# Two fused feed-forward layers behind a window attention: in the unit that ends a layer, the matmuls of the running sums are placed ahead of those of the next product

## The chip, the cores and the metric

The kernel runs on one core of one Trainium2 chip. The metric is the device time of one execution in microseconds, lower is better. Times shown are the median of repeated executions of the same program; one further execution was taken by the hardware profiler, and everything read from a trace comes from that one.

## The reference

```python
w = weight_gen - np.max(weight_gen, axis=-1, keepdims=True)
w = np.exp(w); w = w / (np.sum(w, axis=-1, keepdims=True) + 1e-09)      # softmax over 7 taps
out = np.einsum('bshk,bskhg->bshg', w, x_unf)                           # causal window of 7 tokens, 8 heads
h = x @ w_in;  g = h * np.cos(h);            x = g @ w_out              # layer 1, 192 -> 2048 -> 192
h = x @ w_in2; g = np.maximum(0.01 * h, h);  x = g @ w_out2             # layer 2, 192 -> 2048 -> 192
```

There are 2 x 4096 tokens of 192 numbers, all in float32.

## The kernel before

**Chunks, layers and units.** The 8192 tokens are cut into 16 chunks of 512. For each chunk, layer 1 has 8 units and layer 2 has 8 units; a unit is 256 of the 2048 hidden columns. A unit has a first product (token columns times `w_in`, written into one of three PSUM buffers, the slots), then an activation by ScalarE and VectorE, which leaves the activated values as two parts, `g_hi` and `g_lo`, and then a second product (times `w_out`) that is added to two PSUM accumulators: `acc_a` holds 128 of the 192 result columns, and `acc_b` the other 64 in two halves that are added afterwards. Every factor is split in a high and a low part, so that one product is made of several matmuls.

**How TensorE is fed.** `both_products(i, q, j, r)` (L1215) puts side by side on the two halves of the array (rows 0 to 63 and rows 64 to 127) the first product of unit `q` of chunk `i` and the second product of the unit three before it, `r` of chunk `j`. These are 38 matmuls of 64 rows by 512 columns, issued as 19 pairs: one matmul of each pair on the lower half, one on the upper. Two matmuls that add to the same PSUM buffer from different halves must not overlap, so wherever a buffer changes halves there is a wait. It is for `tiles_done` within a unit, and for `summed` between the units. `summed` is counted up by the last matmul of a unit's second product. The 19 pairs of most units are: 5 pairs that only fill the slot, then, behind a wait for `g_lo` of unit `r` (`lo_ready`) and for `summed` of the unit before (L1250), 14 pairs with the sums in them. The order is written out by hand.

**The last unit of a layer.** Where `r` is the eighth unit of its layer (`v == 7` in the code, `r` 7 or 15), the order differs: `acc_b` gets its last matmul in pair 15 of 19, which counts up `summed_b`, and `acc_a` and the slot get theirs in pair 19.

**Between layers.** When the last unit is through, VectorE copies the upper half of `acc_b` to SBUF and adds the lower half to it (`fold_b` L955, `leave_mid_b` L961 for layer 1, `leave_res_b` L966 for layer 2); it waits for `summed_b`. ScalarE copies `acc_a` out (`leave_mid_a` L756, `leave_res_a` L759); it waits for `summed`. The next unit on TensorE begins the sums of the following layer: behind its 5 filling pairs it waits for both copies (`acc_a_out`, `acc_b_out`, in `wait_to_sum` L1334).

**The activation chain of a unit.** ScalarE copies the activated values to `g_hi` (L730), VectorE subtracts to get `g_lo` (L913), which counts up `lo_ready`. ScalarE's own reads of the slots and the input attention on VectorE lie between.

**Outside the steady part.** The first three units use `fill_alone` (L1352): the 5 filling pairs, a wait for `tiles_done` of the pair just before, and 4 more pairs; so do three others in the second chunk and at the end. `sum_alone` (L1372) does a second product by itself on the whole array; two of them stand right ahead of the last call of `both_products` with `r` 15.

Of the kernel before, what the change touches and what calls it, by code (L numbers as in the profile page):

```python
# [33 lines left out]
FIRST_UNITS = [0, 1, 2, 3, 4, 5, 6, 7]  # L34
# [22 lines left out]
def window_attention_two_ffn(nc, x, weight_gen, w_in1, w_out1, w_in2, w_out2, out):  # L57
# [74 lines left out]
    def unit(i, q):  # L132

        if i == 0:
            return q
        return 8 + 16 * (i - 1) + (q if i < LAST else q - 8)
# [14 lines left out]
    def first_phase(i):  # L151

        return max(0, 2 * i - 1)

    def second_phase(i):
        return 2 * i - (1 if i == LAST else 0)

    ctx = ExitStack()
    with ctx:
# [3 lines left out]
        def sem(name):  # L163
            return ctx.enter_context(nc.semaphore(name))
# [87 lines left out]
        filled = sem("filled")  # L252
        tiles_done = sem("tiles_done")
# [13 lines left out]
        summed = sem("summed")  # L267
        summed_b = sem("summed_b")
# [861 lines left out]
        def _(pe):  # L1130
# [68 lines left out]
            def row_tile_end():  # L1199

                ended[0] += 1
                return ended[0]

            def first_terms(w, x_a_hi, x_a_lo, x_b, f, half):

                c = slice(f * P, (f + 1) * P)
                return [(w.in_a_lo[:, c], x_a_hi), (w.in_a_hi[:, c], x_a_hi),
                        (w.in_a_hi[:, c], x_a_lo), (w.in_b_hi[:, b_columns(half, f)], x_b)]

            def half_product(r, to, w, x, start=False, stop=False):  # L1210

                rows = slice(r * DB, (r + 1) * DB)
                return nc.tensor.matmul(to, w[rows, :], x[rows, :], start=start, stop=stop)  # L1213

            def both_products(i, q, j, r):  # L1215

                w, x_a_hi, x_a_lo, x_b, x_up = operands(q)
                w_then = operands(r)[0]
                u, v, buf = q % 8, r % 8, r % 2
                slot = slots[UNITS[q] % SLOTS]
                P0, P1 = [slot[:, t, :] for t in range(PAIR)]
                A, B = acc_a[:, :], acc_b[:, :]
                b_lo = w.in_b_lo[:, u * P:(u + 1) * P]
                lower, upper = [[first_terms(w, x_a_hi, x_a_lo, x_b, PAIR * u + t, half)
                                 for t in range(PAIR)] for half in range(2)]
                a, b = [], []  # L1230
                for t in range(PAIR):
                    f = PAIR * v + t
                    hi, lo = [g[:, buf, t * N:(t + 1) * N] for g in (g_hi, g_lo)]
                    a_hi, a_lo, b_both = [w_then.out[:, f, c] for c in (
                        slice(0, DA), slice(DA + P, None), slice(DA, DA + P))]
                    a += [(a_hi, hi), (a_hi, lo), (a_lo, hi)]
                    b += [(b_both, hi), (b_both, lo)]

                wait_to_fill(i, q)
                for k in range(4):  # L1240
                    wait_for_tokens(i, q, k)
                    half_product(0, P0, *lower[0][k], start=k == 0)
                    half_product(1, P1, *upper[1][k], start=k == 0)
                half_product(0, P0, b_lo, x_b)
                half_product(1, P1, b_lo, x_up).then_inc(tiles_done, 1)
                first_end = row_tile_end()

                wait_to_sum(j, r)
                if unit(j, r):
                    pe.wait_ge(summed, unit(j, r))  # L1250
                for k in range(4):
                    half_product(0, B, *b[k], start=v == 0 and k == 0)
                    ins = half_product(1, A, *a[k], start=v == 0 and k == 0)
                ins.then_inc(tiles_done, 1)
                sum_b_end = row_tile_end()
                pe.wait_ge(tiles_done, first_end)
                for k in range(2):
                    half_product(0, P1, *lower[1][k])
                    ins = half_product(1, A, *a[4 + k])
                ins.then_inc(tiles_done, 1)  # L1260
                sum_a_end = row_tile_end()
                if v == len(FIRST_UNITS) - 1:
                    pe.wait_ge(tiles_done, sum_b_end)
                    for k in range(2):
                        half_product(0, P1, *lower[1][2 + k], stop=k == 1)
                        half_product(1, B, *b[k])
                    pe.wait_ge(tiles_done, sum_a_end)
                    for k in range(2):
                        half_product(0, A, *a[k])
                        ins = half_product(1, B, *b[2 + k], stop=k == 1)  # L1270
                    ins.then_inc(summed_b, 1)
                    for k in range(4):
                        sum_a = half_product(0, A, *a[2 + k], stop=k == 3)
                        fill_p = half_product(1, P0, *upper[0][k], stop=k == 3)
                    sum_a.then_inc(summed, 1)
                    fill_p.then_inc(filled, 1)
                else:
                    for k in range(2):
                        half_product(0, P1, *lower[1][2 + k], stop=k == 1)
                        half_product(1, P0, *upper[0][k])  # L1280
                    pe.wait_ge(tiles_done, sum_a_end)
                    for k in range(2):
                        half_product(0, A, *a[k])
                        ins = half_product(1, P0, *upper[0][2 + k], stop=k == 1)
                    ins.then_inc(filled, 1)
                    for k in range(4):
                        half_product(0, A, *a[2 + k])
                        ins = half_product(1, B, *b[k])
                    ins.then_inc(summed, 1)
# [19 lines left out]
            def wait_to_fill(i, q):  # L1309
                wait_for_slot(i, UNITS[q])  # L1310
                if i == 0 and q < 8:
                    piece = 0 if q < 2 else 1 if q < 5 else 2
                    pe.wait_ge(w1_hi, 2 * (piece + 1))
                    if q == 0:
                        pe.wait_ge(w1_first_lo, 2)
                    else:
                        pe.wait_ge(w1_lo, 2 * (piece + 1))
                if q == 8 and i == 1:
                    pe.wait_ge(w2_lo, len(W2_PIECES) + 1)

            def wait_for_tokens(i, q, term):

                if q == 0 and term == 0:
                    pe.wait_ge(x1_hi, i * 2 + 1)
                if q == 0 and term == 2:
                    pe.wait_ge(x1_ready, i * 2 + 1)
                if q == 0 and term == 3:
                    pe.wait_ge(x1_ready, i * 2 + 2)
                    pe.wait_ge(x1_up_ready, i + 1)
                if q == 8 and term == 0:  # L1330
                    pe.wait_ge(x2_ready, i * 2)
                    pe.wait_ge(x2_up_ready, i)

            def wait_to_sum(i, q):  # L1334
                if unit(i, q) == 0:
                    pe.wait_ge(unit_dve, 3)
                pe.wait_ge(lo_ready, unit(i, q) + 1)
                if i == 0 and q % 2 == 0:
                    pe.wait_ge(w1_out_lo, q + 2)
                if i == 1 and q >= 8 and q % 2 == 0:  # L1340
                    pe.wait_ge(w2_lo, len(W2_PIECES) + 1 + q - 8 + 2)
                if q in (0, 8) and i > 0:
                    phase = first_phase(i) if q == 0 else second_phase(i)
                    pe.wait_ge(acc_a_out, phase)
                    pe.wait_ge(acc_b_out, phase)

            def operands(q):
                if q < 8:
                    return W1, x1_a_hi, x1_a_lo, x1_b, x1_up
                return W2, x2_a_hi, x2_a_lo, x2_b, x2_up  # L1350
# [29 lines left out]
            def iteration(i):  # L1380
                for q in range(LAG):
                    both_products(i, q, i - 1, q - LAG + len(UNITS))
                for q in range(LAG, len(UNITS)):
                    both_products(i, q, i, q - LAG)
# [25 lines left out]
            for q in range(LAG, 8):  # L1410
                both_products(0, q, 0, q - LAG)
# [47 lines left out]
```

## Time and profile before

| what | value |
|---|---|
| median of 3 executions | 1144.72 us (1144.63 to 1144.95) |
| the profiled execution, its own time | 1145.67 us |
| its span (first to last instruction) | 1143.9 us |
| TensorE matmuls (PE) busy | 1129.4 us, 99% of the span |
| TensorE weight loads (PEld) busy | 996.5 us, 87% |
| VectorE (DVE) busy | 932.0 us, 81% |
| ScalarE (ACT) busy | 723.1 us, 63% |
| GpSimd (POOL) busy | 88.8 us, 8% |
| mean granted TensorE clock | 0.999 |

PE is the matmul side of TensorE, PEld its weight loads, which run beside the matmuls. The start of a matmul is recorded; its end is modelled. Two matmuls of a pair start a few hundredths of a microsecond apart, and each is recorded as 0.39 us long while a new pair starts every 0.227 us, so a busy share of 99% includes overlaps, and small delays have to be read from the distance between starts, not from idle time.

### The profile page before, as it was taken

Reading aid. Unit: us, or ns where it says so; the run is one execution under the profiler, and the core shown is the slowest. Engines: PE = TensorE matmul, PEld = TensorE weight load, DVE = VectorE, ACT = ScalarE, POOL = GpSimd, SP = SyncE. Lnnn points to the kernel's source line nnn. Section 1 sums busy time; section 2 is a strip of 40 time slices with the busy share of each in tenths; the row PEclk is TensorE's granted clock in tenths of the full one; section 3 lists DMA queues with packets and bytes.
Section 4 is the critical chain, followed back from the end, with each engine's and each line's share of the span. In section 5 each row is a group of like instructions: output and inputs, shape, how many; then the busy total and the mean of one; then the engine's idle time right before and its main releaser. Section 6 shows DMA issues by size and latency. Waiting matters only on the chain.

```text
span 1143.9 us, 22933 instructions
## 1 busy us (share of the span) xinstructions
PE 1129.4 (99%) x9766; PEld 996.5 (87%) x9766; DVE 932.0 (81%) x911; ACT 723.1 (63%) x775; POOL 88.8 (8%) x82
## 2 busy tenths in 40 slices
PE   7999999999999999999999999999999999999998
PEld 5778888888988888898888988889899998988986
DVE  7999897988979899697896969879797896978443
ACT  6766775757657576574755757566575655757544
POOL 6860000000000000000000000000000000000000
PEclk9999999999999999999999999999999999999999
DMA  9760201102011110301103011020201102010001
GB/s 256 209 127 1 63 1 40 38 14 64 1 42 36 31 48 1 77 1 36 43 1 77 1 39 40 15 63 1 59 20 32 46 1 77 1 38 6 1 15 29
DMA packets 85262, 48.41 MB, mean 42 GB/s; under 512 B 58156, under 2 KB 78762, under 8 KB 84776
## 3 DMA queue, kind: packets, MB, share of 16 engines
q1 hardware_dynamic: 80712, 41.70, 14.3%
q0 software_dynamic: 4448, 5.24, 2.4%
q8 instruction: 77, 1.26, 0.5%
q14 instruction: 25, 0.20, 0.1%
HBM read 35.12 MB, written 11.80 MB: 41 GB/s over the span
## 4 chain that ended last, share of the span: by engine, by line
PE 91%; DVE 3%; ACT 1%; issue 1%; ACTq 0%
PE slot L1213 42%; PE acc_a L1213 29%; PE acc_b L1213 18%; DVE g_lo L913 1%; DVE gate L1027 1%; ACT gate L793 0%; PE acc_b L1186 0%; PE acc_a L1179 0%; PE acc_b L1187 0%; PE acc_a L1178 0%; PE acc_a L1177 0%; DVE x_a_lo L941 0%; ACT g_hi L730 0%; ACT taps_w L856 0%; DVE gate L908 0%
## 5 line engine op out<-in xcount | busy, mean ns | idle before, releaser
L1213 PE MATMUL acc_a<-g_hi,out_hi_lo 64*128 64x512 f32 x2000 | 696.3, 388 | 0.0
L913 DVE TENSOR_TENSOR g_lo<-gate,g_hi 128x1024 fp32r<-128x1024 f32 x251 | 307.9, 1227 | 121.5 <-ACT g_hi L730 121.4
L1213 PEld LDWEIGHTS acc_a<-g_hi,out_hi_lo 64*128 64x128 f32 x2000 | 367.8, 184 | 26.1
L1213 PE MATMUL acc_b<-g_hi,out_hi_lo 64*128 64x512 f32 x1000 | 388.4, 388 | 1.3 <-DVE g_lo L913 1.2
L1213 PE MATMUL acc_a<-g_lo,out_hi_lo 64*128 64x512 f32 x1000 | 386.5, 386 | 0.0
L1213 PE MATMUL acc_b<-g_lo,out_hi_lo 64*128 64x512 f32 x1000 | 386.4, 386 | 0.0
L730 ACT ACTIVATE g_hi<-gate 128x1024 fp32r<-128x1024 f32 x251 | 266.2, 1061 | 107.7 <-PE acc_b L1213 86.0
L1213 PE MATMUL slot<-x_a_hi,in_a_lo 64*128 64x512 f32 x1024 | 301.0, 388 | 1.6 <-DVE g_lo L927 1.2
L1213 PE MATMUL slot<-x_b,in_b_hi 64*128 64x512 f32 x1024 | 300.6, 387 | 0.5 <-DVE x_b L951 0.2
L1213 PE MATMUL slot<-x_a_lo,in_a_hi 64*128 64x512 f32 x1024 | 300.3, 387 | 0.0
L1213 PE MATMUL slot<-x_a_hi,in_a_hi 64*128 64x512 f32 x1024 | 300.1, 386 | 0.0
L793 ACT ACTIVATE gate<-slot 128x1024 f32<-128x1024 f32 x128 | 130.7, 1021 | 121.6 <-PE slot L1213 95.4
L1213 PEld LDWEIGHTS acc_b<-g_hi,out_hi_lo 64*128 64x128 f32 x1000 | 184.0, 184 | 18.8 <-issue 6.1
L1213 PEld LDWEIGHTS acc_a<-g_lo,out_hi_lo 64*128 64x128 f32 x1000 | 184.2, 184 | 12.0
L1213 PEld LDWEIGHTS acc_b<-g_lo,out_hi_lo 64*128 64x128 f32 x1000 | 184.1, 184 | 9.9
L1027 DVE SCALAR_TENSOR_TENSOR gate<-slot,whole 128x1024 f32<-128x1024 f32 x127 | 155.1, 1221 | 42.4 <-ACT whole L789 41.6
L789 ACT ACTIVATE whole<-slot 128x1024 int32<-128x1024 f32 x127 | 129.9, 1023 | 65.4 <-PE slot L1213 65.4
L1213 PEld LDWEIGHTS slot<-x_a_hi,in_a_lo 64*128 64x128 f32 x1024 | 145.6, 184 | 17.2 <-PE slot L1213 3.0
L1213 PEld LDWEIGHTS slot<-x_b,in_b_hi 64*128 64x128 f32 x1024 | 145.8, 184 | 13.7 <-DVE x_b L944 1.1
L1213 PEld LDWEIGHTS slot<-x_a_lo,in_a_hi 64*128 64x128 f32 x1024 | 145.7, 184 | 12.5 <-DVE x_a_lo L948 0.3
L1213 PEld LDWEIGHTS slot<-x_a_hi,in_a_hi 64*128 64x128 f32 x1024 | 145.7, 184 | 11.6
L908 DVE SCALAR_TENSOR_TENSOR gate<-slot,gate 128x1024 f32<-128x1024 f32 x123 | 150.4, 1223 | 6.1 <-ACT gate L830 4.2
(110 smaller groups left out, 1023.8 us busy)
## 6 DMA issues: line engine op xcount, KB each, us to landing
x_win<-in_x SPq DMA_DIRECT2D x14, 960.0 KB, 4.8
x_columns<-prods SPq DMA_DIRECT2D x56, 96.0 KB, 2.0
out<-turned_a SPq DMA_DIRECT2D x240, 16.0 KB, 1.5
x_raw_a<-x_columns SPq DMA_DIRECT2D x14, 256.0 KB, 2.9
out<-turned_b SPq DMA_DIRECT2D x120, 16.0 KB, 1.5
result<-x_columns SPq DMA_DIRECT2D x14, 128.0 KB, 3.0
out_raw<-in_moe_w_out SPq DMA_DIRECT2D x3, 512.0 KB, 9.7
out_hi_lo<-in_moe_w_out POOLq DMA_DIRECT2D x2, 768.0 KB, 10.2
```

Of the source, the lines that this page charges most:

```text
L730: nc.scalar.activation(g_hi[:, q % 2, :], result_of(i, q), ACT.Copy)\
L789: nc.scalar.activation(whole[:, q % 2, :], slot, ACT.Identity, bias=0.25)\
L793: nc.scalar.activation(gate[:, q % 2, :], slot, ACT.Prelu, alpha=0.01)\
L908: nc.vector.scalar_tensor_tensor(result_of(i, q), slot, RADIANS, gate[:, q % 2, :], ALU.mult, ALU.mult).then_inc(g_ready, 1)
L913: nc.vector.tensor_tensor(g_lo[:, q % 2, :], result_of(i, q), g_hi[:, q % 2, :].bitcast(FP32), ALU.subtract)\
L1027: nc.vector.scalar_tensor_tensor(gate[:, q % 2, :], slot, 0.25, whole[:, q % 2, :], ALU.add, ALU.subtract)\
L1213: return nc.tensor.matmul(to, w[rows, :], x[rows, :], start=start, stop=stop)
```

## The change

In `both_products`, where `r` is the last unit of a layer and not the very first such unit (`unit(j, r) > 7`), another order of the same 38 matmuls is used, and the function returns. There are 30 such calls. The sums' first 4 pairs come first, behind the waits for `lo_ready` and for `summed` of the unit before; then the 5 filling pairs; then 4 pairs with sums alone, of which the last ends `acc_b` (pair 13); then 6 mixed pairs. `acc_a` and the slot still get their last matmul in pair 19. Nothing else is changed: VectorE's, ScalarE's, GpSimd's and the DMA queues' programs are the same row for row.

```diff
+                if v == len(FIRST_UNITS) - 1 and unit(j, r) > v:
+                    wait_to_sum(j, r)
+                    pe.wait_ge(summed, unit(j, r))
+                    for k in range(4):
+                        half_product(0, B, *b[k])
+                        ins = half_product(1, A, *a[k])
+                    ins.then_inc(tiles_done, 1)
+                    sums_end = row_tile_end()
+                    wait_to_fill(i, q)
+                    for k in range(4):
+                        wait_for_tokens(i, q, k)
+                        half_product(0, P0, *lower[0][k], start=k == 0)
+                        half_product(1, P1, *upper[1][k], start=k == 0)
+                    half_product(0, P0, b_lo, x_b)
+                    half_product(1, P1, b_lo, x_up).then_inc(tiles_done, 1)
+                    first_end = row_tile_end()
+                    pe.wait_ge(tiles_done, sums_end)
+                    for k in range(4):
+                        half_product(0, A, *a[k])
+                        ins = half_product(1, B, *b[k], stop=k == 3)
+                    ins.then_inc(summed_b, 1)
+                    pe.wait_ge(tiles_done, first_end)
+                    for k in range(2):
+                        half_product(0, A, *a[4 + k])
+                        ins = half_product(1, P0, *upper[0][k])
+                    ins.then_inc(tiles_done, 1)
+                    sum_a_end = row_tile_end()
+                    for k in range(2):
+                        half_product(0, P1, *lower[1][k])
+                        half_product(1, P0, *upper[0][2 + k], stop=k == 1)
+                    pe.wait_ge(tiles_done, sum_a_end)
+                    for k in range(2):
+                        fill_p = half_product(0, P1, *lower[1][2 + k], stop=k == 1)
+                        sum_a = half_product(1, A, *a[4 + k], stop=k == 1)
+                    sum_a.then_inc(summed, 1)
+                    fill_p.then_inc(filled, 1)
+                    return
```

The first place is TensorE's queue at the start of the last unit of layer 1 in the second chunk (`slot1` is the slot being filled; words in brackets are semaphores that the matmul's weight load waits for). Before:

```order
L1213 MATMUL acc_a<-g_lo,out1_hi_lo 128x512
L1213 MATMUL acc_b<-g_hi,out1_hi_lo 128x512
L1213 MATMUL acc_a<-g_hi,out1_hi_lo 128x512
L1213 MATMUL acc_b<-g_lo,out1_hi_lo 128x512
L1213 MATMUL slot1<-x2_a_hi,in2_a_lo 128x512 [waits g_ready]
L1213 MATMUL slot1<-x2_a_hi,in2_a_lo 128x512
L1213 MATMUL slot1<-x2_a_hi,in2_a_hi 128x512 x2
L1213 MATMUL slot1<-x2_a_lo,in2_a_hi 128x512 x2
L1213 MATMUL slot1<-x2_b,in2_b_hi 128x512 x2
L1213 MATMUL slot1<-x2_b,in2_b_lo 128x512
L1213 MATMUL slot1<-x2_up,in2_b_lo 128x512
L1213 MATMUL acc_b<-g_hi,out1_hi_lo 128x512 [waits summed,lo_ready]
```

In the changed kernel the same place reads:

```order
L1213 MATMUL acc_a<-g_lo,out1_hi_lo 128x512
L1213 MATMUL acc_b<-g_hi,out1_hi_lo 128x512
L1213 MATMUL acc_a<-g_hi,out1_hi_lo 128x512
L1213 MATMUL acc_b<-g_lo,out1_hi_lo 128x512
L1213 MATMUL acc_b<-g_hi,out1_hi_lo 128x512 [waits summed,lo_ready]
L1213 MATMUL acc_a<-g_hi,out1_hi_lo 128x512
L1213 MATMUL acc_b<-g_lo,out1_hi_lo 128x512
L1213 MATMUL acc_a<-g_lo,out1_hi_lo 128x512
L1213 MATMUL acc_b<-g_hi,out1_hi_lo 128x512
L1213 MATMUL acc_a<-g_hi,out1_hi_lo 128x512
L1213 MATMUL acc_b<-g_lo,out1_hi_lo 128x512
L1213 MATMUL acc_a<-g_hi,out1_hi_lo 128x512
```

The wait for `summed` and `lo_ready` stood five pairs behind the matmul that counts `summed` up, and now stands directly behind it.

The second place is TensorE's queue around the last matmul of `acc_b` in the same unit, from there to the unit's end. Before:

```order
L1213 MATMUL acc_a<-g_lo,out1_hi_lo 128x512
L1213 MATMUL acc_b<-g_lo,out1_hi_lo 128x512
L1213 MATMUL acc_a<-g_hi,out1_hi_lo 128x512
L1213 MATMUL slot1<-x2_a_hi,in2_a_lo 128x512
L1213 MATMUL acc_a<-g_hi,out1_hi_lo 128x512
L1213 MATMUL slot1<-x2_a_hi,in2_a_hi 128x512
L1213 MATMUL acc_a<-g_lo,out1_hi_lo 128x512
L1213 MATMUL slot1<-x2_a_lo,in2_a_hi 128x512
L1213 MATMUL acc_a<-g_hi,out1_hi_lo 128x512
L1213 MATMUL slot1<-x2_b,in2_b_hi 128x512
```

In the changed kernel:

```order
L1213 MATMUL acc_b<-g_lo,out1_hi_lo 128x512
L1213 MATMUL acc_a<-g_lo,out1_hi_lo 128x512 [waits tiles_done]
L1213 MATMUL slot1<-x2_a_hi,in2_a_lo 128x512
L1213 MATMUL acc_a<-g_hi,out1_hi_lo 128x512
L1213 MATMUL slot1<-x2_a_hi,in2_a_hi 128x512
L1213 MATMUL slot1<-x2_a_hi,in2_a_lo 128x512
L1213 MATMUL slot1<-x2_a_lo,in2_a_hi 128x512
L1213 MATMUL slot1<-x2_a_hi,in2_a_hi 128x512
L1213 MATMUL slot1<-x2_b,in2_b_hi 128x512
L1213 MATMUL slot1<-x2_a_lo,in2_a_hi 128x512 [waits tiles_done]
L1213 MATMUL acc_a<-g_lo,out1_hi_lo 128x512
L1213 MATMUL slot1<-x2_b,in2_b_hi 128x512
```

Behind the last matmul of `acc_b` there were 4 pairs to the unit's end, and now there are 6 (the first block ends with the unit; of the second only the closing `acc_a` matmul is left out). The next unit's rows are the same in both: 5 filling pairs, then the matmul that waits for `acc_b_out`, `acc_a_out`, `summed` and `lo_ready`.

## Rows read from the trace of the kernel before

**Rows 1.** The page: busy time of each engine (us, share of span, instructions)

```profile
PE 1129.4 (99%) x9766; PEld 996.5 (87%) x9766; DVE 932.0 (81%) x911; ACT 723.1 (63%) x775; POOL 88.8 (8%) x82
```

**Rows 2.** The windows view: stretch, then busy us per engine, granted clock, DMA

```profile
64.60:1095.80 1031.20, 1030.10 (x9040) 921.43 (x9036) 857.92 (x824) 660.08 (x697) 44.98 (x38) 1.00 0.13 31
```

**Rows 3.** The timeline, TensorE, from a middle unit into a last one (start, length)

```profile
308.18 0.39 PE L1213 MATMUL acc_b<-g_lo,out_hi_lo 64*128 64x512 f32 x1
308.35 0.44 PE L1213 MATMUL slot<-x_a_hi,in_a_lo 64*128 64x512 f32 x2
```

**Rows 4.** The timeline, TensorE's matmuls, inside a unit that only fills (near the end)

```profile
1108.79 0.39 PE L1213 MATMUL slot<-x_b,in_b_lo 64*128 64x512 f32 x1
1108.79 0.39 PE L1213 MATMUL slot<-x_up,in_b_lo 64*128 64x512 f32 x1
1109.25 0.50 PE L1213 MATMUL slot<-x_a_hi,in_a_lo 64*128 64x512 f32 x2
1109.59 0.39 PE L1213 MATMUL slot<-x_a_hi,in_a_hi 64*128 64x512 f32 x2
```

**Rows 5.** The timeline, TensorE's weight loads, same place (in brackets: idle before, releaser)

```profile
1109.25 0.19 PEld L1213 LDWEIGHTS slot<-x_a_hi,in_a_lo 64*128 64x128 f32 x2 [0.50 <-PE slot L1213]
1109.36 0.19 PEld L1213 LDWEIGHTS slot<-x_a_hi,in_a_hi 64*128 64x128 f32 x2
```

**Rows 6.** The timeline, VectorE: g_lo of two last units

```profile
272.42 1.22 DVE L913 TENSOR_TENSOR g_lo<-gate,g_hi 128x1024 fp32r<-128x1024 f32 x1
...
305.45 1.23 DVE L913 TENSOR_TENSOR g_lo<-gate,g_hi 128x1024 fp32r<-128x1024 f32 x1
```

**Rows 7.** The timeline, TensorE, the start of the last unit at 273.77

```profile
273.56 0.39 PE L1213 MATMUL acc_b<-g_lo,out_hi_lo 64*128 64x512 f32 x1
273.77 0.40 PE L1213 MATMUL slot<-x_a_hi,in_a_lo 64*128 64x512 f32 x2
```

**Rows 8.** The timeline around 1101, last call with r 15: TensorE, then VectorE

```profile
1101.01 0.50 PE L1213 MATMUL slot<-x_a_hi,in_a_lo 64*128 64x512 f32 x2
1101.35 0.40 PE L1213 MATMUL slot<-x_a_hi,in_a_hi 64*128 64x512 f32 x2
...
1100.42 1.23 DVE L913 TENSOR_TENSOR g_lo<-gate,g_hi 128x1024 fp32r<-128x1024 f32 x1
```

**Rows 9.** The timeline, between the layers at 312: all engines

```profile
312.10 0.69 DVE L958 COPY fold<-acc_b 64x512 f32<-64x512 f32 x1 [0.76 <-PE acc_b L1213]
...
312.65 0.44 PE L1213 MATMUL slot<-x_a_hi,in_a_lo 64*128 64x512 f32 x2
...
312.83 0.68 DVE L963 TENSOR_TENSOR mid_b<-acc_b,fold 64x512 f32<-64x512 f32 x1
312.85 0.60 ACT L757 ACTIVATE mid_a<-acc_a 128x512 f32<-128x512 f32 x1 [3.13 <-PE acc_a L1213]
...
317.07 0.41 PE L1213 MATMUL slot<-x_a_hi,in_a_lo 64*128 64x512 f32 x2
```

**Rows 10.** The timeline, behind layer 2 at 486: VectorE, ScalarE, TensorE

```profile
486.18 0.85 DVE L976 TENSOR_TENSOR res_b<-acc_b,fold 64x256 f32<-64x256 f32 x2
...
486.34 0.60 ACT L764 ACTIVATE res_a<-acc_a 128x512 f32<-128x512 f32 x1 [1.82 <-PE acc_a L1213]
...
486.15 0.40 PE L1213 MATMUL slot<-x_a_hi,in_a_lo 64*128 64x512 f32 x2
...
490.57 0.44 PE L1213 MATMUL slot<-x_a_hi,in_a_lo 64*128 64x512 f32 x2
```

**Rows 11.** The waits: who waited for whom, us in total, times, longest

```profile
DVE fold L958 <- PE acc_b L1213: 26.0, 30, 3.1
PEld acc_b L1213 <- issue: 6.1, 29, 0.5
```

**Rows 12.** The timeline, TensorE, the slowest start of a layer's sums

```profile
174.44 0.39 PE L1213 MATMUL slot<-x_b,in_b_lo 64*128 64x512 f32 x1
...
174.96 0.46 PE L1213 MATMUL acc_b<-g_hi,out_hi_lo 64*128 64x512 f32 x1
```

## The prediction

> **What bounds the kernel now.** I read the page first. TensorE's matmuls are busy for 99% of the span, VectorE for 81%, ScalarE for 63% [rows 1]. The windows view says the same of the steady part alone: from 64.6 to 1095.8 us PE is busy for 1030.10 of 1031.20 us at a granted clock of 1.00, the upper of its two levels, 2.4 GHz [rows 2]. So the time is the number of pairs times the distance between their starts, plus the places where that distance is longer. Since ends of matmuls are modelled, idle time does not show these places, and I went to the timeline and measured starts. A pair follows the one before after 0.227 us, and a unit of 19 pairs takes 4.30 us: in rows 3 a last unit starts at 308.35 and in rows 9 its successor starts at 312.65. A change that only reorders matmuls can therefore gain no more than the delays that stand in the timeline now, and it loses whatever it adds to the distance between two pairs.
>
> **What the change can gain.** Each layer's sums start behind a wait for the two copies of the old accumulators. In rows 9 ScalarE's copy of `acc_a` runs from 312.85 to 313.45, VectorE's work on `acc_b` ends at 312.83 + 0.68 = 313.51, so `acc_b` is the last by 0.06 us. The unit that waits there takes 317.07 - 312.65 = 4.42 us, which is 0.12 over a plain unit. Behind layer 2 `acc_b` is through at 486.18 + 0.85 = 487.03 and `acc_a` at 486.94 [rows 10]; that unit takes 490.57 - 486.15 = 4.42 us, again 0.12 over. The waits view counts 29 such starts, where the weight load of the first sum stood idle for 6.1 us in all [rows 11]. That idle time is an upper figure, since part of it is there without any wait; 29 times 0.12 is 3.5 us, and this is what I take as the delay.
>
> The new order ends `acc_b` two pairs earlier, 2 x 0.227 = 0.45 us. VectorE can use it: it was idle 26.0 us ahead of its 30 copies of `acc_b`, 0.87 us each on the mean and 0.76 in rows 9 [rows 9, 11]. So `acc_b` stops being the last. What is late next is `acc_a`. Its last matmul stays in pair 19, ScalarE's copy still takes 0.60 us, and it ends only 0.06 to 0.09 us ahead of today's last. I take that 0.07 of the 0.12 goes and 0.05 stays. One start was slower than the others: the first sum came 174.96 - 174.44 = 0.52 us behind the last filling pair instead of 0.227 [rows 12], and with 0.45 us more cover I expect nearly all of the extra 0.3 to go. The gain is 29 x 0.07 + 0.3, some **2.3 us**. Its bounds are nothing (if `acc_a` alone sets these starts) and 29 x 0.12 + 0.3 = 3.8 us (if all delays go).
>
> **What the change costs.** The new first matmul of a last unit waits for `summed` of the unit before. That semaphore is counted up by the very matmul that now stands directly ahead of it, where before five filling pairs, 1.13 us, lay between and hid it. On TensorE everything queues behind that weight load, the filling pairs too, and both halves of the array run dry. The kernel of before has the same pattern in one place: a unit that only fills waits for the pair just issued. There the pair starts at 1108.79 and ends at 1109.18, and the next weight load and its matmul start at 1109.25 [rows 4, 5]. That is 0.46 us from start to start in place of 0.227. The pair behind it also comes late, at 1109.59, 0.34 us on, because its weights could only be loaded from 1109.36 [rows 5]; of the 0.34, 0.227 is the plain distance. So one such wait costs (0.46 - 0.227) + (0.34 - 0.227) = 0.23 + 0.11 = **0.34 us**. In rows 4 the two matmuls of the pair start together. In rows 3 the second starts at 308.18, 0.06 behind the first (308.35 - 0.227 = 308.12), so its end and the semaphore would come 0.06 later, and the price is 0.39 to 0.40. In rows 7 the same reckoning gives only 0.02. Since a drained array starts both halves together, I take 0.34 for all.
>
> There are 30 calls. In 29 of them nothing else is later: `g_lo` of the last unit, now wanted 1.13 us earlier, is ready at 305.45 + 1.23 = 306.68 where the unit starts at 308.35 [rows 3, 6]. In the tightest place that I found it is ready at 272.42 + 1.22 = 273.64, while the `summed` wait lets the load go only at about 273.56 + 0.39 + 0.06 = 274.01, where 0.06 is the distance from the modelled end to the load in rows 4 and 5 [rows 4 to 7]. So 29 x 0.34 = **9.9 us**. The thirtieth is the last call, at 1101.01. There the preceding matmuls run on the whole array, and `g_lo` is only ready at 1100.42 + 1.23 = 1101.65 [rows 8]. The unit would start at about 1101.71 instead of 1101.01, with the same 0.34 to the second pair as now, so it adds **0.7 us**; half of it might be given back by later waits, and a rather later start costs 0.9.
>
> The three waits for `tiles_done` within the new unit lie five, four and two pairs behind what they wait for. Today's lie four and two behind (the code at L1215 and below), and the last unit that starts in rows 3 takes the plain 4.30 us with them in it, so they cost nothing. The filling pairs and their wait for a free slot come 4 pairs later, which can only relax it. The slot is filled in pair 19 as before, so ScalarE's and VectorE's next reads keep their distance. Every TensorE delay gives these engines slack, and they have the same rows to do.
>
> **The sum.** 9.9 + 0.7 - 2.3 = **+8.3 us**. Against the profiled execution, 1145.67 us, that is 1154.0; the median of the runs shown is 0.95 lower, and against it I say **1153.0 us**. The bounds: 29 x 0.33 + 0.4 - 3.8 = +6.2 and 29 x 0.40 + 0.9 - 0 = +12.5, so 1150.9 to 1157.2. About 0.2%, 2.3 us, is what a measurement of this kernel tells from no change, and the change is well over it.
>
> **The rivals.** *Faster: the new wait is hidden.* Break-even is at (2.3 - 0.7) / 29 = 0.055 us per wait. If the queue covered the `summed` wait to less than that, only the gain would be left: 1144.72 - 2.3 + 0.7 = 1143.1, or 1142.4 without the late `g_lo`. For it: the same `summed` wait costs nothing in all units now. Against it: there five pairs stand between, and where none does the trace shows 0.34 us [rows 4]. Chance 0.04.
>
> *Half price: the second pair is not late.* If the second pair's weights were in place when the first may start, the 0.11 would fall away: 29 x 0.23 + 0.7 - 2.3 = +5.1, so 1149.8. Against it: rows 4 and 5 show the second pair's load starting 0.11 behind the first's. Chance 0.06. The Trainium skill, page "TensorE: Matmul & The Clock Gate", section "Part 2: What happens when you issue a matmul", says that TensorE may pull weight loads ahead of matmuls in flight where the row groups don't conflict; by that rule the upper half's load would not stand behind the lower half's wait, and the sum would come out nearer this rival. This trace shows the loads of both halves held until the wait ends [rows 5], and I go by the row.
>
> *More: other waits appear.* Each layer change holds TensorE up for a third of a microsecond, and the activation chain may fall out of step so that `g_lo` is late in some of the 29, by up to the 0.7 of the last call. If it were in every third, 10 x 0.7 more, +15, some 1160. Against it: a delay on TensorE leaves this chain's work the same and its time longer. Chance 0.06.
>
> *No change within the bound.* It needs the new wait at about 0.05 to 0.1 us and the whole gain; 1144.7. Chance 0.03.
>
> **How the numbers follow.** The forecast has 0.81. The range takes its bounds and the half-price rival's neighbourhood: 1150.4 to 1157.2. Faster by over 0.2%: 0.04; within: 0.03; slower: 0.93.
>
> **What would show it.** Right: in the timeline, at the 30 last units the first sum's pair starts 0.45 to 0.46 us behind the pair before and the next one 0.34 us on; the waits view has a new row of about 29 waits of `acc_b`'s weight load for PE, some 0.5 us of idle each; last units take 4.64 us. `fold` starts about 0.45 us earlier against the end of its unit, `acc_b`'s copy ends before `acc_a`'s, and units behind a layer change take 4.35 rather than 4.42 us. Wrong: last units at 4.30 us (first rival), at 4.53 (second), or a row of `acc_b`'s weight load waiting for `g_lo` with more than a few entries (third).

## The result, and the profile after

The changed kernel is **slower**: 1155.95 us (median of 6, 1155.28 to 1156.38) against 1144.88 us (median of 6), a ratio of 1.0096 with a 95% interval of 1.0086 to 1.0106. That is 11.1 us. The prediction said 1153.0 us and a range up to 1157.2. The two profiled executions lie 10.3 us apart (spans 1143.9 and 1154.2 us), since the one of before took 0.8 us more than its median. All executions compared below ran at a granted clock of 0.998 or more; one of summed_on_load ran at 0.557 and took 1910.78 us, and the ratios leave it out.

The page and the windows view, changed kernel, as in [rows 1] and [rows 2]:

```profile
PE 1135.2 (98%) x9766; PEld 940.4 (81%) x9766; DVE 935.1 (81%) x911; ACT 721.9 (63%) x775; POOL 88.0 (8%) x82
```

```profile
64.60:1107.00 1042.40, 1036.92 (x9048) 865.86 (x9045) 860.37 (x825) 659.95 (x700) 44.85 (x38) 1.00 0.12 31
```

The clock is still 1.00, and VectorE and ScalarE do what they did. PE has 5.5 us of idle in the steady part (1042.40 - 1036.92) where it had 1.1, and since ends of matmuls are modelled, even that hides more than half of the loss. The busy share of the weight loads fell from 87 to 81%, but it does not measure the loss: two_fills_first below, as fast as the kernel before, has 82%. It follows how far the two loads of a pair overlap: their lengths add up to 1768 us in both kernels, and the matmuls of a pair start 0.06 us apart at [rows 3] and 0.00 to 0.03 us apart in the lines below.

The timeline of TensorE's matmuls, changed kernel, where a last unit of layer 1 begins (start, length; at the same point of a unit as [rows 3]):

```profile
519.88 0.39 PE L1213 MATMUL acc_b<-g_hi,out_hi_lo 64*128 64x512 f32 x1
520.11 0.39 PE L1213 MATMUL acc_a<-g_hi,out_hi_lo 64*128 64x512 f32 x1
520.11 0.39 PE L1213 MATMUL acc_b<-g_lo,out_hi_lo 64*128 64x512 f32 x1
520.65 0.47 PE L1213 MATMUL acc_b<-g_hi,out_hi_lo 64*128 64x512 f32 x1 [0.15 <-PE acc_b L1213]
520.65 0.50 PE L1213 MATMUL acc_a<-g_hi,out_hi_lo 64*128 64x512 f32 x1
520.96 0.39 PE L1213 MATMUL acc_b<-g_lo,out_hi_lo 64*128 64x512 f32 x1
520.99 0.39 PE L1213 MATMUL acc_a<-g_lo,out_hi_lo 64*128 64x512 f32 x1
```

The unit's first pair starts 0.54 us behind the pair before it (520.11 to 520.65), where 0.227 is plain, and the next one 0.31 to 0.34 later. The same pattern stands at all 29 last units, 0.54 us each time. The waits view of the changed kernel, answering to [rows 11] (total, times, longest):

```profile
PEld acc_b L1213 <- issue: 14.2, 26, 0.5
PE acc_b L1213 <- PE acc_b L1213: 4.5, 29, 0.2
DVE fold L958 <- PE acc_b L1213: 26.0, 30, 3.3
```

The second row is new. The first has the name of a row of [rows 11] but holds other places: there it was the 29 starts of a layer's sums, and here it is 26 of the 29 last units, 0.55 us each. The other three last units, with the same 0.55 us, are put down to `g_lo`; it was no later there than elsewhere, since their distances are the same.

The timeline at the layer change behind that unit, all engines, as in [rows 9] (weight loads left out):

```profile
524.02 0.69 DVE L958 COPY fold<-acc_b 64x512 f32<-64x512 f32 x1 [0.74 <-PE acc_b L1213]
...
524.75 0.68 DVE L963 TENSOR_TENSOR mid_b<-acc_b,fold 64x512 f32<-64x512 f32 x1
...
525.08 0.39 PE L1213 MATMUL slot<-x_a_hi,in_a_lo 64*128 64x512 f32 x2
...
525.31 0.60 ACT L757 ACTIVATE mid_a<-acc_a 128x512 f32<-128x512 f32 x1 [3.65 <-PE acc_a L1213]
...
526.00 0.40 PE L1213 MATMUL slot<-x_up,in_b_lo 64*128 64x512 f32 x1
...
526.23 0.39 PE L1213 MATMUL acc_b<-g_hi,out_hi_lo 64*128 64x512 f32 x1
```

The intended half of the change works. `fold` starts 1.06 us ahead of the next unit's first matmul, where in [rows 9] it was 0.55. `acc_b` is through at 525.43, half a microsecond ahead of `acc_a` (525.91), and the first sum follows the last filling pair after a plain 0.23 us. That next unit ends here (timeline, TensorE):

```profile
529.42 0.40 PE L1213 MATMUL slot<-x_a_hi,in_a_lo 64*128 64x512 f32 x2
```

It takes 529.42 - 525.08 = 4.34 us, 0.03 over a plain unit, where it was 0.12 over. The last call with `r` 15, answering to [rows 8] (TensorE, then VectorE):

```profile
1110.40 0.40 PE L1179 MATMUL acc_a<-g_hi,out_hi_lo 128*128 128x512 f32 x1
1111.39 0.50 PE L1213 MATMUL acc_b<-g_hi,out_hi_lo 64*128 64x512 f32 x1 [0.59 <-DVE g_lo L913]
...
1110.11 1.23 DVE L913 TENSOR_TENSOR g_lo<-gate,g_hi 128x1024 fp32r<-128x1024 f32 x1
```

`g_lo` ends at 1111.34 and the sums start 0.05 us later.

To put all places on one scale, I took from each trace the distance between the first matmuls of successive units and subtracted the plain 19 x 0.2267 us. The column "last unit" is the extra time of one of the 29, the piece in front of its first matmul and the piece behind it; "29 starts" is the sum over the units in which a layer's sums begin.

| kernel | median us | last unit, each | last call | 29 starts, sum |
|---|---|---|---|---|
| before (first trace) | 1144.88 | 0.00 | 0.00 | 3.70 |
| changed | 1155.95 | 0.315 + 0.125 = 0.44 | +0.68 | 0.86 |

The changed kernel's books close: 29 x 0.44 + 0.68 - (3.70 - 0.86) = +10.6 us, against 10.3 us between the two spans.

### The profile page after: what moved, and what is told of

It is laid out like the page before. It is cut to its first block, busy times and chain, and to the rows that moved or that the text cites. A ratio compares the mean times of both kernels' runs of the same rounds, so it can differ in the third digit from the quotient of the medians.

```text
span 1154.2 us, 22933 instructions
## 1 busy us (share of the span) xinstructions
PE 1135.2 (98%) x9766; PEld 940.4 (81%) x9766; DVE 935.1 (81%) x911; ACT 721.9 (63%) x775; POOL 88.0 (8%) x82
## 4 chain that ended last, share of the span: by engine, by line
PE 90%; DVE 3%; issue 1%; ACT 1%; ACTq 0%
PE slot L1213 42%; PE acc_a L1213 29%; PE acc_b L1213 18%; DVE g_lo L913 1%; DVE gate L1027 1%; ACT gate L793 0%; PE acc_b L1186 0%; ACT g_hi L730 0%; DVE x_a_lo L1000 0%; DVE x_a_lo L941 0%; ACT taps_w L856 0%; DVE gate L908 0%; DVE x_b L944 0%; PE acc_a L1179 0%; PE acc_b L1187 0%
## 5 line engine op out<-in xcount | busy, mean ns | idle before, releaser
L1213 PE MATMUL slot<-x_a_hi,in_a_lo 64*128 64x512 f32 x1024 | 297.4, 388 | 1.6 <-DVE g_lo L927 1.2
L1213 PE MATMUL slot<-x_b,in_b_hi 64*128 64x512 f32 x1024 | 296.9, 387 | 0.6 <-DVE x_b L951 0.2
L1213 PE MATMUL slot<-x_a_hi,in_a_hi 64*128 64x512 f32 x1024 | 296.5, 387 | 0.0
L1213 PE MATMUL slot<-x_a_lo,in_a_hi 64*128 64x512 f32 x1024 | 296.5, 387 | 0.0
L1213 PEld LDWEIGHTS slot<-x_a_hi,in_a_lo 64*128 64x128 f32 x1024 | 142.5, 184 | 22.4 <-PE slot L1213 2.9
L1213 PEld LDWEIGHTS slot<-x_b,in_b_hi 64*128 64x128 f32 x1024 | 142.1, 184 | 20.1 <-DVE x_b L944 1.1
L1213 PEld LDWEIGHTS slot<-x_a_lo,in_a_hi 64*128 64x128 f32 x1024 | 142.3, 184 | 18.6 <-DVE x_a_lo L948 0.2
L1213 PEld LDWEIGHTS slot<-x_a_hi,in_a_hi 64*128 64x128 f32 x1024 | 142.4, 184 | 17.4
L830 ACT ACTIVATE gate<-gate 128x1024 f32<-128x1024 f32 x127 | 134.5, 1059 | 32.6 <-DVE gate L1027 31.2
```

Source lines behind the costliest of these rows:

```text
L830: nc.scalar.activation(gate[:, q % 2, :], gate[:, q % 2, :], ACT.Sin, scale=TURN).then_inc(cos_ready, 1)
```

## The experiments

Some split the loss from the gain, some move the wait, some ask what the gain is made of, and two repeat a kernel. Executions of one kernel differ by about 2 us, and a trace shows only one of them: that of three_fills_first is the fastest of its ten (1141.68 us), that of three_fills_told_late the slowest of its eleven (1145.32 us). Sums read from traces are therefore rougher than the medians.

**summed_on_load.** The two waits ahead of the first sum change places, and with that the weight load carries the wait for `summed`; a wait instruction ahead of it in the queue carries the one for `g_lo`. In the changed kernel it is the other way round.

```diff
-                    wait_to_sum(j, r)
                     pe.wait_ge(summed, unit(j, r))
+                    wait_to_sum(j, r)
```

> The changed kernel with the two waits ahead of the first sum of a last unit in the other order, so that the wait for summed is carried by the weight load itself and the one for g_lo by a wait instruction of the queue ahead of it. Theory A: the new wait cost 0.44 us in place of 0.34 because summed was waited for by a separate queue instruction (0.05 us long) with the weight load behind it; here the load starts about 0.045 us behind the semaphore as in the units that only fill, the first pair comes 0.46 to 0.47 us behind the one before instead of 0.54, and the run takes 29 x 0.08 = 2.3 us less than the changed kernel, 1153.6 us. Rival B: the extra comes from the accumulators themselves (both halves write the buffers that they swap), not from the form of the wait: the distance stays 0.54 and the time 1155.9 us.

It took 1154.03 us, a ratio to before of 1.0078 (1.0064 to 1.0091), 1.9 us under the changed kernel. It was run again for a trace:

> summed_on_load once more for its trace, whose first profile was taken at half the clock. Theory A: the first sum's pair of a last unit starts 0.46 to 0.47 us behind the pair before, against 0.54 in the changed kernel, and the time is near 1154.0 us. Rival B: 0.54 us, and the time differs for another reason.

1153.74 us (ratio 1.0076, 1.0053 to 1.0099). The timeline, TensorE's matmuls, of that second run:

```profile
519.27 0.38 PE L1213 MATMUL acc_a<-g_hi,out_hi_lo 64*128 64x512 f32 x1
519.28 0.39 PE L1213 MATMUL acc_b<-g_lo,out_hi_lo 64*128 64x512 f32 x1
519.73 0.49 PE L1213 MATMUL acc_b<-g_hi,out_hi_lo 64*128 64x512 f32 x1
519.73 0.49 PE L1213 MATMUL acc_a<-g_hi,out_hi_lo 64*128 64x512 f32 x1
520.06 0.39 PE L1213 MATMUL acc_b<-g_lo,out_hi_lo 64*128 64x512 f32 x1
```

0.46 us to the first pair, 0.33 to the second: 0.225 + 0.134 = 0.36 us each, nearly the 0.34 of [rows 4]. Theory A holds. The buffers are the same, so the form of the wait made the 0.08 us. The last call pays in turn: there `g_lo` is what it waits for, now through the queue instruction, and its extra time went up by 0.06 us.

**acc_b_told_late.** The changed order, but VectorE hears of `acc_b` from a matmul of pair 15.

```diff
-                    ins.then_inc(summed_b, 1)
                     pe.wait_ge(tiles_done, first_end)
                     for k in range(2):
-                        half_product(0, A, *a[4 + k])
+                        late = half_product(0, A, *a[4 + k])
                         ins = half_product(1, P0, *upper[0][k])
+                    late.then_inc(summed_b, 1)
```

> The changed kernel, but VectorE is told of the end of acc_b two pairs later (by a matmul of pair 15, where it stood in the kernel before); TensorE's order is the changed one. Theory A: ending acc_b early is worth about 0.1 us at each of 29 starts of a layer's sums (0.028 us of delay left against 0.12 to 0.15 before), so this run loses 2.9 us: 1158.8 us, and VectorE's part of acc_b ends last again. Rival B: the shorter delays at those starts come from ScalarE and VectorE having more time behind the new wait, not from acc_b: the time stays 1155.9 us.

1157.59 us (1.0112, 1.0097 to 1.0127), 1.6 us more than the changed kernel. The timeline between the layers, VectorE and ScalarE:

```profile
525.82 0.68 DVE L963 TENSOR_TENSOR mid_b<-acc_b,fold 64x512 f32<-64x512 f32 x1
525.95 0.60 ACT L757 ACTIVATE mid_a<-acc_a 128x512 f32<-128x512 f32 x1 [3.65 <-PE acc_a L1213]
```

`acc_b` is through at 526.50 and `acc_a` at 526.55, so the half microsecond is gone. The 29 starts cost 2.37 us again instead of 0.86. Theory A has the direction, but its size, 2.9 us, was too large: the starts don't go back to 3.70. One reason shows in the lines: `acc_b` is through 0.05 us before `acc_a` here, where in [rows 9] it was 0.06 behind, so the edit does not put VectorE back quite to where it was. The start in the third chunk returns in full, 0.39 us where the changed kernel has 0.06.

**wait_alone.** The order of before, with the wait for `summed` also ahead of the filling pairs.

```diff
+                if v == len(FIRST_UNITS) - 1 and unit(j, r) > v:
+                    pe.wait_ge(summed, unit(j, r))
                 wait_to_fill(i, q)
```

> The kernel before, its order kept, with one edit: the wait for summed of the unit before also stands ahead of the five filling pairs in the same 30 units. Theory A: a wait directly behind the matmul that it waits for costs 0.34 to 0.36 us each where the load carries it (here it does), and nothing is gained: 1144.9 + 29 x 0.35 = 1155.0 us (1157.7 if it is the 0.44 of the changed kernel). Rival B: the cost lies in the new order of sums and filling pairs, and the wait is nearly free: 1144.9 us.

1157.05 us (1.0109, 1.0095 to 1.0122). The timeline, TensorE's matmuls, then its weight loads:

```profile
520.57 0.39 PE L1213 MATMUL acc_a<-g_hi,out_hi_lo 64*128 64x512 f32 x1
...
521.02 0.50 PE L1213 MATMUL slot<-x_a_hi,in_a_lo 64*128 64x512 f32 x2
521.36 0.39 PE L1213 MATMUL slot<-x_a_hi,in_a_hi 64*128 64x512 f32 x2
```

```profile
521.02 0.18 PEld L1213 LDWEIGHTS slot<-x_a_hi,in_a_lo 64*128 64x128 f32 x2 [0.48 <-PE acc_b L1213]
521.13 0.19 PEld L1213 LDWEIGHTS slot<-x_a_hi,in_a_hi 64*128 64x128 f32 x2
```

One wait costs 0.224 + 0.149 = 0.37 us, with nothing else moved: rival B is out, the place of the wait makes the loss. The span, 1154.1 us, fits that. The time is 1 us longer than the span lets one expect: its profiled execution took 1156.95 us, 2.9 around the span (its four executions have 1.9 to 2.9), where the other kernels have 1.8. What that microsecond is stays open.

**two_fills_first.** Two filling pairs ahead of the sums' four pairs, three behind. `acc_b` still ends behind pair 13.

```diff
+                    wait_to_fill(i, q)
+                    ahead = 2
+                    for k in range(ahead):
+                        fill_pair(k)
                     wait_to_sum(j, r)
                     pe.wait_ge(summed, unit(j, r))
                     for k in range(4):
                         half_product(0, B, *b[k])
                         ins = half_product(1, A, *a[k])
                     ins.then_inc(tiles_done, 1)
                     sums_end = row_tile_end()
-                    wait_to_fill(i, q)
-                    for k in range(4):
...
+                    for k in range(ahead, 5):
+                        fill_pair(k)
```

> The changed kernel, with two of the five filling pairs ahead of the sums' first four pairs and three behind them. acc_b still ends behind pair 13, but the wait for summed stands two pairs behind its matmul, and the sums' change of halves three pairs behind. Theory A: the whole loss is the wait's place, and the gain of 3.3 us stays: 1144.9 - 3.3 = 1141.6 us; last units take 4.31 us and units behind a layer change 4.34 us. The last call, where g_lo is late, loses little, since two pairs cover 0.45 us or more of its 0.65. Rival B: two pairs (0.45 us) are too few for a semaphore that comes 0.41 us behind and a queue instruction of 0.05 us with the load behind it: some 0.1 us is left at each, and the time is 1144.5 us. Rival C: without the new wait the early acc_b is worth nothing: 1144.9 us.

1144.04 us (0.9992, 0.9983 to 1.0001), 11.9 us less than the changed kernel: the loss is gone, and the kernel is not clearly faster than the one before. That is 2.4 us over what theory A said and nearer to rival B's 1144.5, though not by its reason: 0.02 us is left at each wait, not 0.1. Each last unit keeps 0.023 us (0.7 in all), the 29 starts cost 1.24 us, and one unit, at 195 us, waited 0.29 us for its input. The 3.3 us of gain in the expectation was also read from the first trace of before, which is slow at these starts (see before_again).

**one_fill_first.** The same with `ahead = 1`.

> As two_fills_first, but one filling pair ahead and four behind. Theory A (the price is the part of 0.44 us that the pairs between do not cover): 0.44 - 0.227 = 0.21 us at each of 29 last units in place of 0.023, so 29 x 0.19 = 5.5 us over two_fills_first, 1149.5 us. Rival B (a wait that is reached at all costs a fixed piece, by draining the queue): 0.3 us or more each, 1152 us or more.

1148.44 us (1.0029, 1.0017 to 1.0040). The timeline, TensorE's matmuls:

```profile
517.33 0.39 PE L1213 MATMUL acc_a<-g_hi,out_hi_lo 64*128 64x512 f32 x1
517.34 0.39 PE L1213 MATMUL acc_b<-g_lo,out_hi_lo 64*128 64x512 f32 x1
517.56 0.39 PE L1213 MATMUL slot<-x_a_hi,in_a_lo 64*128 64x512 f32 x2
517.88 0.47 PE L1213 MATMUL acc_b<-g_hi,out_hi_lo 64*128 64x512 f32 x1
517.88 0.49 PE L1213 MATMUL acc_a<-g_hi,out_hi_lo 64*128 64x512 f32 x1
518.18 0.39 PE L1213 MATMUL acc_b<-g_lo,out_hi_lo 64*128 64x512 f32 x1
```

The first sum's pair starts 0.54 us behind the last pair of the unit before (517.34 to 517.88), exactly as in the changed kernel; one filling pair is done meanwhile. Each unit pays 0.20 us, which is 0.44 less one pair of 0.227, as theory A had it. The whole is 4.4 us over two_fills_first where 5.5 were expected; rival B, 1152 us or more, is out.

**two_fills_on_load.** two_fills_first with the exchange of summed_on_load.

> two_fills_first with the order of the two waits exchanged, so that the weight load carries the wait for summed. Theory A: the semaphore comes 0.41 us behind, the load may start 0.045 us later, at 0.455, and two pairs are 0.454: the 0.023 us at each of 29 last units goes, 0.7 us less than two_fills_first. Rival B: the 0.023 us is not from the wait: no difference.

1143.05 us (0.9983, 0.9974 to 0.9991), 1.0 us less, and the last units are at 0.00, as theory A said. Its last call costs 0.06 more. Its 29 starts, which the edit does not touch, cost 0.39 us instead of 1.24; why is not shown.

**three_fills_first.** `ahead = 3`, two filling pairs behind the sums.

> As two_fills_first, but three filling pairs ahead of the sums' first four and two behind them. Theory A (a distance decides): the wait for summed lies three pairs (0.68 us) behind its matmul, more than the 0.41 us of the semaphore and the 0.1 us of the queue's instruction and load, so the 0.023 us that two pairs left at each of 29 last units goes; the sums' change of halves lies two pairs behind its matmul with the load carrying the wait, which costs nothing elsewhere; the last call loses 0.2 us less. 0.7 + 0.2 under two_fills_first: 1143.1 us. Rival B (two pairs are too few for the change of halves in this order): the last units show a delay behind pair 9 and the time is 1144 us or more.

**1142.73 us** (0.9978, 0.9969 to 0.9987), faster than both kernels. The timeline, TensorE's matmuls, at the start of a last unit:

```profile
514.61 0.39 PE L1213 MATMUL acc_b<-g_lo,out_hi_lo 64*128 64x512 f32 x1
514.83 0.40 PE L1213 MATMUL slot<-x_a_hi,in_a_lo 64*128 64x512 f32 x2
...
515.28 0.40 PE L1213 MATMUL slot<-x_a_lo,in_a_hi 64*128 64x512 f32 x2
515.51 0.39 PE L1213 MATMUL acc_b<-g_hi,out_hi_lo 64*128 64x512 f32 x1
515.52 0.39 PE L1213 MATMUL acc_a<-g_hi,out_hi_lo 64*128 64x512 f32 x1
515.74 0.39 PE L1213 MATMUL acc_b<-g_lo,out_hi_lo 64*128 64x512 f32 x1
```

Every distance is 0.23 us. At its layer change, all engines:

```profile
518.81 0.68 DVE L963 TENSOR_TENSOR mid_b<-acc_b,fold 64x512 f32<-64x512 f32 x1
...
519.37 0.60 ACT L757 ACTIVATE mid_a<-acc_a 128x512 f32<-128x512 f32 x1 [3.21 <-PE acc_a L1213]
...
520.04 0.39 PE L1213 MATMUL slot<-x_b,in_b_lo 64*128 64x512 f32 x1
...
520.27 0.39 PE L1213 MATMUL acc_b<-g_hi,out_hi_lo 64*128 64x512 f32 x1
```

`acc_a` is through at 519.97, 0.30 us ahead of the first sum at 520.27, and TensorE does not wait: the 29 starts cost 0.27 us in all. The last call costs nothing more than before.

**three_fills_told_late.** The same, and VectorE told late as in acc_b_told_late.

> three_fills_first, but VectorE is told of the end of acc_b two pairs later (by a matmul of pair 15, where it stood before). It measures what ending acc_b early is worth where no new wait stands in the way. Theory A: the delay at the starts of a layer's sums goes from 0.04 back to 0.12 and 0.09 us, and the slow start in the third chunk comes back with 0.35 us: 29 x 0.065 + 0.35 = 2.2 us over three_fills_first. Rival B (the gain came from the order of the last pairs, which leaves both halves of the array starting together): under 1 us over it.

1144.66 us (0.9997, 0.9988 to 1.0006), 1.9 us over three_fills_first: theory A. The 29 starts cost 2.18 us instead of 0.27, 0.38 us of it in the third chunk. So by the medians 1.9 of the 2.2 us that the improved order wins come from VectorE hearing earlier of `acc_b`. The traces leave the order of the matmuls a part too: the 29 starts cost 2.18 us here and 3.18 or 3.70 in the kernel before, and the last units give half a microsecond of that back, 0.02 us each. Nor is VectorE told quite as late as before: `fold` starts 0.63 us ahead of the next unit here and 0.55 in [rows 9].

**acc_a_waited_first.** The kernel before with its own order of matmuls; only the two waits at the start of a layer's sums change places.

```diff
                 if q in (0, 8) and i > 0:
                     phase = first_phase(i) if q == 0 else second_phase(i)
-                    pe.wait_ge(acc_a_out, phase)
                     pe.wait_ge(acc_b_out, phase)
+                    pe.wait_ge(acc_a_out, phase)
```

The name tells the order in TensorE's queue, and there it is the reverse of the program's text: of these two waits the one written second (L1345) is the first instruction in the queue, in both kernels.

The reason to try it stands in the trace of before, at the layer change of [rows 9], where `acc_b` is through at 313.51. These are the queue's two wait instructions there, each by its line (shortest, middle and longest duration in ns; start of the first and last), and the first weight load from the timeline. The first is the wait for `acc_b`; the second, at L1250, carries the waits for `acc_a` and `summed`:

```profile
L1345 PEldq EVENT_SEMAPHORE  x1: 51/51/51, 313.5 to 313.5; - x1
```

```profile
L1250 PEldq EVENT_SEMAPHORE  x1: 51/51/51, 313.7 to 313.7; - x1
```

```profile
313.74 0.18 PEld L1213 LDWEIGHTS acc_b<-g_hi,out_hi_lo 64*128 64x128 f32 x1 [0.16 <-issue]
```

The semaphore that comes last is waited for first, and the other instruction and the load follow one by one: 0.2 us from 313.51 to 313.74. In three_fills_first, at the layer change shown above, the same two instructions and the load stand so:

```profile
L1393 PEldq EVENT_SEMAPHORE  x1: 51/51/51, 519.5 to 519.5; - x1
```

```profile
L1298 PEldq EVENT_SEMAPHORE  x1: 365/365/365, 519.6 to 519.6; - x1
```

```profile
520.05 0.18 PEld L1213 LDWEIGHTS acc_b<-g_hi,out_hi_lo 64*128 64x128 f32 x1
```

The wait for `acc_b` is through at 519.6, and the second instruction stands waiting until `acc_a` is there at 519.97; the load follows 0.08 us later.

> The kernel before, with one edit: where a layer's sums begin, the waits for acc_a_out and acc_b_out change places. In the traces the two waits are two queue instructions of 0.05 us, 0.11 us apart, with the weight load 0.08 us behind the second; before, acc_b's stands first, and acc_b is ready last, so all of the 0.19 us comes behind it. Theory A: the 0.12 us of delay at these 29 starts is this chain of instructions behind the last semaphore, and what the changed orders gained by ending acc_b early is that its instruction is done ahead. With acc_a's first (0.06 to 0.09 us earlier) the load comes 0.06 to 0.08 us sooner: 29 x 0.07 = 2.0 us less, 1142.9 us, without touching the order of the matmuls. Rival B: the delay is VectorE's lateness itself, and the instructions run ahead: no difference, 1144.9 us.

**1142.95 us** (0.9979, 0.9969 to 0.9988): by the ratio 1.4 to 3.5 us less than before, where theory A said 2.0, and as fast as three_fills_first within the intervals. Rival B is out. Most starts fall to 0.02 us of delay; the one in the third chunk keeps 0.29. So what the earlier `acc_b` bought, outside the third chunk, was mainly a queue instruction that is through before `acc_a` comes. The new order and this exchange were not run together.

**before_again.** The kernel before, for a second trace.

> The kernel before, once more, for a second trace: its first profiled execution took 0.8 us more than its median. If the starts of a layer's sums cost 3.5 us in both, the gain that the prediction counted has the right base; if they cost under 2.5 us here, the base was too large in the first trace.

1144.57 us, one execution. Its 29 starts cost 3.18 us, where the first trace has 3.70. The base in the prediction (3.5 plus 0.3) was in the right place and somewhat large; against this trace the changed kernel gained 2.3 us at the starts, against the first 2.8.

| kernel | median us | last unit, each | last call | 29 starts, sum |
|---|---|---|---|---|
| before_again | 1144.57 | 0.00 | +0.02 | 3.18 |
| summed_on_load_again | 1153.74 | 0.36 | +0.74 | 0.61 |
| acc_b_told_late | 1157.59 | 0.41 to 0.44 | +0.69 | 2.37 |
| wait_alone | 1157.05 | 0.37 | +0.16 | 3.16 |
| one_fill_first | 1148.44 | 0.20 | +0.45 | 1.17 |
| two_fills_first | 1144.04 | 0.02 | +0.23 | 1.24 |
| two_fills_on_load | 1143.05 | 0.00 | +0.29 | 0.39 |
| three_fills_first | 1142.73 | 0.00 | 0.00 | 0.27 |
| three_fills_told_late | 1144.66 | 0.02 | +0.03 | 2.18 |
| acc_a_waited_first | 1142.95 | 0.00 | 0.00 | 1.12 |

## Why the prediction was right, and where its sizes were off

**The new wait.** The mechanism was right: a wait directly behind the matmul that it waits for drains both halves of the array. wait_alone shows it by itself, and the series with none, one, two and three filling pairs between (0.44, 0.20, 0.02, 0.00 us) shows that the price is what the pairs between do not cover, to within 0.02 us. What was off is the term "29 x 0.34": it measured 0.44, which is 29 x 0.10 = 2.9 us. The price was taken from [rows 4], where the weight load itself waits. In the changed kernel the weight load has a second wait, for `g_lo`, and the one for `summed` stands in a queue instruction ahead of it. summed_on_load brought the first distance back to 0.46 us and the price to 0.36. The order listing had shown both waits at that matmul, and the prediction did not ask which of them came last and who carried it. The bounds that it gave the term, 0.33 to 0.40, miss the 0.44 as well. That the time still fell inside the range is owed to the other term: the upper bound counted no gain at all, and with 0.44 for each wait and no gain the sum would have been 13.4 us, over the 12.5 of the bound.

**The last call.** 0.7 us forecast, 0.68 measured, by the step that the prediction gave: `g_lo` ends, and the sums start 0.05 us later.

**The gain.** 2.3 us forecast. The step "0.07 of the 0.12 goes and 0.05 stays" was somewhat cautious: 0.03 stays in the changed kernel, so it gained 2.3 to 2.8 us, depending on which trace of before is the base. The reason given for the rest, that `acc_a` is late next, fell. `acc_a` is out 0.83 us behind the start of the unit in the changed kernel and in three_fills_first, no earlier than the 0.80 of [rows 9], and yet only 0.03 and 0.01 us are left per start. In the kernel before, `acc_b` was later than `acc_a` by only 0.01 to 0.09 us at 28 of the 29 starts; the rest of the delay was the second wait instruction behind it, as acc_a_waited_first shows, and it went too. The slow start in the third chunk went as forecast (0.44 to 0.06 us), and came back in both kernels in which VectorE is told late.

**The rest.** The waits for `tiles_done` cost nothing, as said; three_fills_first has the sums' change of halves two pairs behind, and its units are plain. `g_lo` was late at no other last unit, so the rival with further waits did not come. Its sign in the waits view, `acc_b`'s weight load waiting for `g_lo`, has 8 entries instead of 4, but three of them are the last units that lose the same 0.55 us as the rest. The half-price rival is out as well, since the second pair was late at each of the 29. The Trainium skill, "TensorE: Matmul & The Clock Gate", section "Part 2: What happens when you issue a matmul", lets weight loads be pulled ahead where the row groups don't conflict. These traces do not show that past a wait: in wait_alone the loads of both halves stand at 521.02 us, behind it.

## What to carry to other kernels

A wait is priced by what is queued between it and the instruction that ends it: here a semaphore of TensorE's own cost 0.44 us directly behind its matmul and nothing three pairs behind, so work that doesn't depend on it belongs between the two. If one buffer should end earlier for another engine, look for an order that ends it at the same pair and keeps a few independent pairs in front; here it turned 11 us of loss into 2 us of gain. Where several waits meet at one instruction, look in the trace for the one that comes last and let it be the last one in the queue, best on the instruction itself; exchanging two lines won as much as the best reordering.

## What the runs showed of the hardware that I had not expected

- The same wait cost 0.36 us where the weight load carried it and 0.44 us where a queue instruction ahead of the load did (first distance 0.46 and 0.54 us), and exchanging two lines of the program was enough to move it: 1.9 and 2.2 us of 1155.95 in two runs.
- Several waits in front of one weight load are gone through one by one, some 0.11 us apart, even when all but the first have been met: at 313.5 us `acc_a` had been out for 0.06 us when `acc_b` came, and the load still started 0.22 us behind `acc_b` (313.74), against 0.08 us behind `acc_a` in three_fills_first. Exchanging them was worth 2 us in 29 places.
- `fold` behind layer 1 of the third chunk starts 0.36 us later against its unit than elsewhere (in the changed kernel 0.69 instead of 1.06 us ahead of the next unit), in each trace, though VectorE is idle ahead of it. It is not the semaphore: in the trace of before the wait instruction ahead of it (L957) starts at 172.84 us and takes 0.05 us, and `fold` starts at 173.30. What holds it up stays open.
